# A fused attention and two feed-forward layers on one core: each attention unit's outputs moved to the place of the next unit's scores

## What is computed

```python
q_d, k_d, v_d = (a.reshape(B, H, S // 4, 4, D).mean(axis=3) for a in (q, k, v))
out_up = np.repeat(sm_attn(q_d, k_d, v_d), 4, axis=2)
scores = np.where(abs(i - j) < 4, scale * q @ k.T, -1e9)
x = out_up + softmax(scores) @ v                     # then (2304, 512)
x = (silu(x @ w_gate) * (x @ w_val)) @ w_out         # 512 -> 1536 -> 512
h = x @ w_in                                         # 512 -> 2048 -> 512
return (np.maximum(h, 0) + alpha * np.minimum(h, 0)) @ moe2_w_out
```

## Time and profile before

| | before |
|---|---|
| median of 3 runs | 945.27 us (945.24 to 945.83) |
| the profiled execution's own time | 944.62 us |
| its span in the profile | 942.6 us |
| TensorE matmul busy | 925.4 us, 98% |
| TensorE weight load busy | 819.2 us, 87% |
| VectorE busy | 503.9 us, 53% |
| ScalarE busy | 275.3 us, 29% |
| GpSimd busy | 138.9 us, 15% |

### The profile page before, as it was taken

How to read it: one execution, slowest core, us unless ns; L and a number is a source line. 1 busy time by engine, 2 the same in 40 slices (tenths; PEclk the granted TensorE clock), 3 DMA queues, 4 the chain that set the end, 5 groups by cost and what they waited for, 6 DMA issues and landing times.

```text
span 942.6 us, 18796 instructions
## 1 busy us (share of the span) xinstructions
PE 925.4 (98%) x7752; PEld 819.2 (87%) x7752; DVE 503.9 (53%) x951; ACT 275.3 (29%) x692; POOL 138.9 (15%) x167
## 2 busy tenths in 40 slices
PE   4999999999999999999999999999999999999998
PEld 3899999999999998888899999888888888888886
DVE  8799777545466765453334555444444344444343
ACT  5665444322233433222224432111112111111111
POOL 7876011000011000000016530000000000000000
PEclk9999999999999999999999999999999999999999
DMA  9763323211122222100044430100020020001001
GB/s 271 248 206 98 111 82 103 85 50 41 42 82 97 81 72 86 41 22 14 1 134 134 135 102 1 67 1 0 4 87 1 1 89 2 0 1 45 1 1 45
DMA packets 30691, 63.21 MB, mean 67 GB/s; under 512 B 3344, under 2 KB 10768, under 8 KB 30608
## 3 DMA queue, kind: packets, MB, share of 16 engines
q1 hardware_dynamic: 30608, 62.02, 20.6%
HBM read 52.57 MB, written 9.44 MB: 66 GB/s over the span
## 4 chain that ended last, share of the span: by engine, by line
PE 89%; DVE 1%; issue 0%; ACT 0%; DVEq 0%; ACTq 0%
PE ps L1114 50%; PE ps L1159 21%; PE ps L1142 14%; PE ps L1062 1%; PE ps L998 1%; PE ps L1008 1%; PE ps L1075 1%; PE ps L1046 1%; ACT turned_one L616 0%; DVE v_d_one L784 0%; DVE hidden L946 0%; DVE x_lo L851 0%; DVE y_sb L984 0%; DVE row_max L810 0%; ACT down L598 0%
## 5 line engine op out<-in xcount | busy, mean ns | idle before, releaser
L688 ACT CAST h_hi<-hidden 128x512 fp32r<-128x512 f32 (+4 forms) x152 | 83.2, 548 | 417.9 <-DVE hidden L966 328.1
L1114 PE MATMUL ps<-x_hi,w_hi 128*128 128x416 f32 (+3 forms) x573 | 198.4, 346 | 0.2 <-issue 0.2
L1114 PE MATMUL ps<-x_lo,w_hi 128*128 128x416 f32 (+3 forms) x573 | 192.6, 336 | 0.0
L1114 PE MATMUL ps<-x_hi,w_lo 128*128 128x416 f32 (+3 forms) x573 | 192.5, 336 | 0.0
L930 DVE TENSOR_TENSOR h_lo<-hidden,h_hi 128x512 fp32r<-128x512 f32 (+4 forms) x152 | 109.5, 720 | 67.8 <-ACT h_hi L688 67.8
L963 DVE TENSOR_SCALAR gated<-ps,alpha_sb 128x512 f32<-128x512 f32 (+1 forms) x80 | 55.8, 698 | 162.2 <-PE ps L1114 162.2
L1114 PEld LDWEIGHTS ps<-x_hi,w_hi 128*128 128x128 f32 x573 | 107.6, 188 | 6.6 <-issue 0.5
L1159 PE MATMUL ps<-w_hi,h_hi 128*128 128x512 f32 x288 | 112.2, 390 | 0.0
L1159 PE MATMUL ps<-w_hi,h_lo 128*128 128x512 f32 x288 | 112.2, 390 | 0.0
L1159 PE MATMUL ps<-w_lo,h_hi 128*128 128x512 f32 x288 | 112.0, 389 | 0.0
L1114 PEld LDWEIGHTS ps<-x_hi,w_lo 128*128 128x128 f32 x573 | 107.7, 188 | 4.1
(11 more groups left out here) (141 smaller groups left out, 1341.4 us busy)
## 6 DMA issues: line engine op xcount, KB each, us to landing
w_home<-w SPq DMA_DIRECT2D x68, 256.0 KB, 4.0
qk<-qk SPq DMA_DIRECT2D x30, 436.0 KB, 3.9
vsrc_one<-vsrc SPq DMA_DIRECT2D x58, 144.0 KB
vwin<-vwin SPq DMA_DIRECT2D x30, 192.0 KB, 2.4
x_raw<-y_t SPq DMA_DIRECT2D x4, 1024.0 KB, 6.6
out<-y_sb SPq DMA_DIRECT2D x3, 1024.0 KB, 5.5
y_t<-y_sb SPq DMA_DIRECT2D x2, 832.0 KB, 4.5
y_t<-y_sb SPq DMA_DIRECT2D x2, 576.0 KB, 3.9
```

Of the source, the lines that this page charges most:

```text
L688: nc.scalar.copy(h_hi[r][:, 0:width], hidden[r][:, 0:width]).then_inc(h_hi_ready, 1)
L1114: mm = nc.tensor.matmul(out_ps, w[:, piece, 128 * k:128 * k + 128], x_parts[low][:, k, :], start=(k == 0 and n == 0), stop=(k == KC - 1 an ...
```

## The change

The change does three things.

1. **Places.** `SLOTS_IN` names 29 places. At each, TensorE makes the scores of one unit and, right behind them, the outputs of the unit before (at the first place scores alone, at the last outputs alone). Transposes stand one place ahead of the outputs at the latest, `turn_local` in the same place. `add_up` stands two places behind the outputs, and `x_lo` three; where the outputs fall into the last three places of a block, they stand at the outputs' place and one behind (`due`). `average_v` stands three places behind the scores. There are now 13 units scored in blocks 0 and 1 where there were 12.
2. **PSUM.** Transposes and outputs lie in columns from 256 on (`OUT_AT`) of banks 6 and 7, beside the scores' 240. Waits go with it: the mask waits for the outputs of the unit before (`att_ready`), the scores for the copy of its transposes (`down_copied`), `add_up` for the scores behind its outputs.
3. **Casts and prologue.** In block 0 ScalarE casts a place's weight piece ahead of that place's attention. In the prologue GpSimd averages the values of units 1 and 3 where it did 2 and 3, VectorE those of 0 and 2, and ScalarE's copies of transposes stand ahead of `x_hi`.

```diff
-SCORED_IN = ((1, 7, 13, 19, 25, 31), (1, 6, 11, 17, 22, 27), (2, 10, 18, 26), (0, 4, 8, 12, 16, 20, 25, 29), (2, 10, 18, 26))
+SLOTS_IN = ((1, 7, 13, 19, 25, 31), (1, 6, 12, 17, 23, 28, 34), (4, 13, 22, 31), (0, 5, 10, 15, 20, 25, 29, 34), (5, 14, 23, 31))
...
+    def __init__(self, q, scored, put_out, narrow):
+        apart = put_out - scored
+        self.q, self.scored, self.put_out = q, scored, put_out
+        self.exponentials = self.next_averaged = scored + 1
+        self.summed = scored + 2
+        self.v_averaged = scored + 3
+        self.flipped = scored + (4 if narrow and apart > 5 else 3)
+        self.turned = self.transposed = min(self.flipped + 1, put_out - 1)
+        self.due = put_out % PLACES > PLACES - 4
+        self.added = put_out if self.due else put_out + 2
+        self.split = self.added + 1
...
-            average_v(2)
+            average_v(1)
             normalise(2, 2, 0)
...
             turn_local(0, 2, 0)
+            copy_down_t(0, 2, 0)
             split_x_hi(0, 0, 0)
-            copy_down_t(0, 2, 0)
             turn_local(0, 3, 0)
+            copy_down_t(0, 3, 0)
             split_x_hi(0, 1, 0)
-            copy_down_t(0, 3, 0)
+            split_x_hi(0, 2, 0)
             first_weights_hi(2)
-            split_x_hi(0, 2, 0)
...
-                        attention(PLACES * j + p)
                         piece = EARLY_PIECES + p
                         if not j and piece < P1:
                             first_weights_hi(piece)
+                        attention(PLACES * j + p)
...
                 dve.wait_ge(scores_ready, q + 1)
+                if mode:
+                    dve.wait_ge(att_ready, q)
...
                 if mode:
-                    pe.wait_ge(x_added, outputs_before)
-                    pe.wait_ge(shifted, q)
-                    pe.wait_ge(down_ready, q)
+                    pe.wait_ge(x_added, q - 1 if q > PAIRS else PAIRS)
+                    pe.wait_ge(down_copied, q)
...
-            average_v(0, 1)
             reciprocals(0, 3, 0)
             flip_local(0, 2, 0)
             add_up(0, 0, 0)
             flip_local(0, 3, 0)
+            average_v(0, 2)
```

More of the change, by code:

```diff
@@ L51 @@
 DOWN_O = HALF_Q
+OUT_AT = 256
 TOKENS, DM = BATCH * SEQ, HEADS * HEAD
@@ L109, in schedule @@
-def schedule():
[L110 to L121, removed]
+    def __init__(self, q, scored, put_out, narrow):
[9 more added lines that the diff above has]
+        self.split = self.added + 1
@@ L124 @@
+def schedule():
+    slots = [PLACES * b + p for b, places in enumerate(SLOTS_IN) for p in places]
+    return [Unit(PAIRS + n, slots[n], slots[n + 1], SPANS[slots[n] // PLACES] == TB) for n in range(UNITS - PAIRS)]
 WORK = schedule()
@@ L700, in attention @@
                         turn_local(a, k, 1)
-                    if g == unit.put_out + 1:
+                for unit in WORK:
+                    a, k = divmod(unit.q, PAIRS)
+                    if g == unit.split:
                         split_x_hi(a, k, 1)
@@ L838, in add_up @@
                 dve.wait_ge(att_ready, q + 1)
+                if mode:
+                    dve.wait_ge(scores_ready, min(q + 2, UNITS))
                 if not mode and k:
@@ L907, in attention @@
                     a, k = divmod(unit.q, PAIRS)
-                    if g == unit.put_out:
+                    if g == unit.added and unit.due:
                         add_up(a, k, 1)
+                for unit in WORK:
+                    a, k = divmod(unit.q, PAIRS)
                     if g == unit.scored:
@@ L916, in attention @@
                         flip_local(a, k, 1)
-                    if g == unit.put_out + 1:
+                for unit in WORK:
+                    a, k = divmod(unit.q, PAIRS)
+                    if g == unit.added and not unit.due:
+                        add_up(a, k, 1)
+                    if g == unit.split:
                         split_x_lo(a, k, 1)
@@ L1064, in pair_outputs @@
                                              start=True, stop=True)
-                if mode or k < POOL_AVERAGES:
+                if mode:
                     pe.wait_ge(v_averaged, q + 1)
+                elif k % 2:
+                    pe.wait_ge(v_averaged_pool, k // 2 + 1)
                 else:
-                    pe.wait_ge(v_averaged_pool, k - POOL_AVERAGES + 1)
+                    pe.wait_ge(v_averaged, k // 2 + 1)
                 for c in range(2):
@@ L1098, in attention @@
                     a, k = divmod(unit.q, PAIRS)
+                    if g == unit.transposed:
+                        transpose_down(a, k, 1)
+                for unit in WORK:
+                    a, k = divmod(unit.q, PAIRS)
                     if g == unit.scored:
-                        pair_scores(a, k, a % 2, 1, unit.outputs_before)
-                    if g == unit.transposed:
-                        transpose_down(a, k, 1, unit.overlapped, unit.outputs_between)
+                        pair_scores(a, k, a % 2, 1)
+                for unit in WORK:
+                    a, k = divmod(unit.q, PAIRS)
                     if g == unit.put_out:
```

38 lines of the change are left out of this document (20 added, 18 removed).

## The result

The change made the kernel slower: a median of 957.14 us over 4 runs (955.78 to 957.30) against 945.25 over 4 runs of the kernel before. The ratio is 1.0123, with an interval of 1.011 to 1.0135, so +11.9 us. The forecast was 953.2 with a range up to 956.5: the sign and the mechanism came out, the size fell short by 3.9, and the time lies 0.6 above the range. One execution among the experiments, the profiled one of the kernel with the casts behind attention, took 1139.67 at a mean granted clock of 0.76, and no reading rests on it.

The account below looks back on a forecast made before the run. TensorE, its matmuls busy 98% of the span, was taken as the bound, with VectorE nearly deciding in block 0. Terms -4.2 + 11.6 - 0.4 - 0.2 + 1.1 = +7.9 gave a median of 953.2 us, range 943.0 to 956.5.

Parts of the forecast that it names:

- the held `x_lo`: Block 0: GpSimd's pair of `w_lo` starts just ahead of `x_lo` and holds it to 4.22 us behind the reciprocal's start.
- the ring: Block 0: outputs, mask, sums, `row_inv`, flip, `turn_local` and outputs again form a closed chain with a period of 15.2 us.
- Joined places, -4.2: Behind place 37: 21 joined places each save one entering and leaving of attention, 0.20 us, giving -4.2.
- Block 0, +11.6: Places 7 to 37: three periods of 15.2, one 14.7, one 11.57; sum 71.9 us against 60.3 before.
- outputs 0.76 with a hop of 0.08 at each side: Block 0's last link, from `turn_local` done at 8.35 us behind the reciprocal's start to the next mask at 9.2.
- The race: Block 0: whether GpSimd's `w_lo` pair or VectorE's `x_lo` starts first; the pair forecast ahead by 0.05 us.
- rival 1: Block 0: `x_lo` is issued ahead of the pair, 2.35 us less in each of four periods, 943.8; chance 0.22.
- Prologue, -0.4: Third transposes at 19.1 us for 20.84, first product some 27.1 for 29.04; lead 0.4 by the end of place 7.
- Block 1, -0.2: GpSimd rests; chain of 9.7 us covered by TensorE's 10.0 for five places; one old `turn_local` wait ends, saving 0.2.
- block 2's start, +1.1: Unit 15's outputs at place 70: steps to `x_lo` take 4.4 us against 3.3 of products, costing 1.1.
- In blocks 2 to 4 a place is 2.3 and longer: covered.: Places there last 2.3 us or more, so the chain between outputs was forecast to cost TensorE nothing.
- What would show it: Signs listed for the later timeline: `x_lo` over 2 us, `neg_max` 0.8 or more, mask to mask 15, joined places 1.80.

Follow-up runs that it names:

- the old prologue: The kernel with the late piece, its prologue put back as before the change (GpSimd averaging values 2 and 3, old ScalarE and VectorE orders): 942.13 us, ratio 0.9964.
- the late piece: Changed kernel with casts behind attention, `x_lo` first, `due` `x_hi` and later `v_d` moved ahead, each unit's last `w_lo` piece behind its normalisation: 941.09 us, ratio 0.9957.
- the late waits alone: Changed kernel, block 0 untouched, with `v_d` ahead of `x_lo` from block 1 on and `x_hi` ahead of the exponentials for `due` units: 953.76 us, ratio 1.0095.
- the gap: Changed kernel with each of GpSimd's `w_lo` pieces in block 0 waiting until the one before is done: 949.58 us, ratio 1.0045.

## Why the prediction was right and where it was wrong

The sum was +7.9 and the spans give +12.7. The path and the held `x_lo` were right; three terms were too small, and together they carried the time out of the range: the outputs at the end of the ring, sized at the full clock; the prologue, taken as a gain of 0.4; and place 137, put at nothing. Step by step:

- **Joined places, -4.2.** Right. The saving was an estimate between 0 and 0.20 with 0.20 taken; the places of block 1 show 0.17 to 0.24 (1.77 to 1.80 for 1.97 to 2.01). TensorE's busy time hides it, since the matmuls are the same.
- **Block 0, +11.6: the mechanism right, the size short by 1.7.** The four periods sum to 61.97 for a forecast of 60.3. By the steps: mask to reciprocal 5.92, 6.22, 5.92, 5.97 for 6.0 each, so nothing in sum. Reciprocal to the end of `turn_local` 8.32, 8.35, 8.33 for 8.35 in the first three. What is left is the last link, "outputs 0.76 with a hop of 0.08 at each side": 9.94, 9.36, 9.80 and 8.84 for 9.2, 9.2, 9.2 and 8.7. In the first and third of these the outputs ran at a granted clock of 0.5, which costs 0.57 of the first (1.33 for 0.76). The term was sized at the full clock, though the sum itself put an idle of some 3 us ahead of these matmuls. In the other two, at the full clock, the link from `turn_local`'s end to the mask is 1.01 and 1.02 for 0.92, so the hops are 0.1 longer. And 8.35 + 0.08 + 0.76 + 0.08 is 9.27, not the 9.2 that the sum used, which makes 0.3 over the four.
- **The race.** The forecast put it at 0.45 against 0.22 for the rival that `x_lo` is issued first, on a margin of 0.05. The margin was 0.01 and the outcome the same in all four periods. Part of this is cause and part luck. The cause: `x_hi`, which stands ahead of `x_lo`, and the cast that the pair needs are both ScalarE's, and casting first had the pair ready in time; with the cast behind, GpSimd waits 0.54 for it and loses the race. The prediction counted that part of the change only by `neg_max` (1.0) and by a cast on ScalarE's path (0.5), 5.5 us in four periods, where the undo of it gave 9.0. The sum was not wrong for it, since it had the held `x_lo` in a term of its own. The luck: with the cast ready, the pair starts 1.37 behind the reciprocal and `x_lo` 1.38, at the end of two chains that have nothing else in common, and rows that give 0.05 could not tell which comes first.
- **Contention as the cause.** Shown: letting `x_lo` go first, with GpSimd's work as it is, gives 10.6, of which rival 1 had 9.4 (943.8 from 953.2), and with memsets for GpSimd's `w_lo` the periods are 11.70 (941.56). That rival's time, 943.8, was low by 2.8, since it took its 9.4 from a sum that lacked the terms below.
- **Prologue, -0.4: wrong by 1.3.** The transposes were forecast at 19.1 for 20.84; they started at 20.48. `average_v` for unit 1 now runs on GpSimd from 16.07 to 17.11, right behind a normalisation, and VectorE's `first_neg` takes 1.22 until 17.13, where it took 0.22 before; GpSimd then waits for the reciprocal that stands behind it. (The same work stood 0.35 later already at 12 us, ahead of anything that was changed on GpSimd.) The timeline of VectorE, GpSimd and TensorE:

```profile
15.91 1.22 DVE L814 TENSOR_SCALAR first_neg<-first_max 72x2 f32<-72x2 f32 x1
...
16.07 1.04 POOL L558 TENSOR_TENSOR vsrc_early<-vsrc_early 100x512 f32<-100x512 f32 x1
...
19.30 0.51 POOL L546 TENSOR_TENSOR local_early<-local_early,first_inv 128x192 f32<-128x192 f32 x1 [1.46 <-DVE first_inv L827]
...
20.48 0.72 PE L1052 MATMUL ps<-ident,down_early 72*100 72x72 f32 x4 [1.15 <-POOL down_early L549]
```

  So the first product of L1126 came at 28.83, 0.2 earlier than before and not 1.9. Then the products from 32.16 to 34.80 ran at the lower clock, 12 of them some 0.11 longer, 1.3 in all, where before that stretch had a clock of 1.00. The end of place 7 came 0.9 later than before for a forecast of 0.4 earlier (43.93 for 41.73, less 1.27 for the transposes and outputs that now stand ahead of it). Not every kernel here has this slow stretch: the one with the old prologue does not, nor the one with the late piece, nor the one with the late waits alone, whose program is the same up to there. What decides it wasn't tried, so the 1.3 is read from one profile.
- **Block 1, -0.2, and block 2's start, +1.1.** The second measured 1.03. The end of place 37, counted like that of place 7, stood 14.2 later than before (117.49 for 102.06, less 1.27) for a forecast of 11.2; the 3.0 of difference are the two terms above. Counted the same way, block 1 itself comes to about 0, not -0.2.
- **"In blocks 2 to 4 a place is 2.3 and longer: covered."** Wrong at one place of them, 137, by some 1.55: 1.35 of wait and the hops around it. The rule that covers the units was right by the length of the places, but the unit with four places between scores and outputs has a queue in its way: `v_d` behind `x_lo` behind `x_hi` behind `turn_local`. It was named in no rival.
- **What would show it.** Of the signs, `x_lo` over 2 us, `neg_max` at 0.8 or more in two of the four (1.16, 0.52, 1.17, 0.63), the waits, mask to mask, and 1.80 for a joined place came as written. Scores wait for `down_t_one` more than outputs for `turned_one`, as forecast by their order.

Terms of the difference between 7.9 and 12.7: prologue and place 7 +1.3, block 0 +1.7, place 137 +1.55, and 0.25 left, of which block 1 is some 0.2. The range missed by 0.6 because its upper end came from a longer ring alone, and took in neither a slower TensorE nor a second place that waits.

## What to carry to other kernels

When a change makes a chain close on itself within a few places, work out its period link by link, and read for each link whether another engine reads SBUF at that moment; an instruction on two or eight columns counts as much as a large one (here up to 1.17 and 1.19 for 0.17). Whether a held instruction goes first or last can hang on the order of two unrelated ones on a third engine: look at what gates the neighbour (here one weight cast) and set that order, rather than trust a margin of hundredths. And give a new idle of TensorE its price twice: the wait itself, and the matmuls behind it at the lower clock where they are on the chain.

## What the runs showed of the hardware

- A VectorE instruction on two SBUF tensors waits while GpSimd reads, but for how many of GpSimd's instructions is not settled here. `x_lo` was held through both of a pair in all four periods of the changed kernel (2.85 for 0.46, ending 0.3 behind the pair). It got in behind the first where the second waited for the first's end (1.60, four of four). But without such a wait and with no idle shown, `x_lo` got in behind the first in one of four periods with `v_d` ahead (0.66), and `h_lo` behind the second of three pieces in the kernel with the late piece (0.92), where the next piece took 1.49 for 1.27.
- An instruction of 2 columns (0.17 alone) took up to 1.17, one of 8 columns (0.17) up to 1.19, while GpSimd read two tensors. Beside GpSimd's memset, which reads nothing, `x_lo` took 0.46 as it does alone, but `row_padded` took 0.32 and ended 0.02 behind the memset.
- TensorE's granted clock stood at 0.5 (1.2 GHz) right behind an idle of 3.34 and some 1.2 behind the end of one of 3.35, and at 1.00 behind those of 2.33 and 1.86, in the changed kernel. But with `v_d` ahead, two waits of 2.20 were followed by 0.50 (57 to 59 and 84 to 85), and with the gap one of 1.79 by 0.50 (97 to 99), so the length of the idle alone doesn't give the answer. No experiment changed the idle alone.
